# Attention by whole batches in 32-column tiles, with long-run loads, inside a fused attention and MoE kernel

## The reference

```python
def sm_attn(qq, kk, vv):
    s = scale * np.matmul(qq, kk.transpose(0, 1, 3, 2))
    s = s - np.max(s, axis=-1, keepdims=True)
    a = np.exp(s)
    a = a / (np.sum(a, axis=-1, keepdims=True) + 1e-09)
    return np.matmul(a, vv)
p_packed = sm_attn(p, k, v)            # 32 rows attend to 576
out = sm_attn(q, p_packed, p_packed)   # 576 rows attend to 32
...
k = np.maximum(xk @ w_k, 0.0); v = k * k @ w_v        # 512 -> 1024 -> 512
r = 1.0 / (1.0 + np.exp(-(xr @ w_r)))                 # xk, xr: x mixed with its previous row
x = r * v
...
u = x + (x^T @ U @ V)^T
out = u + np.maximum(u @ w_ch1, 0.0) @ w_ch2          # 512 -> 2048 -> 512
```

## Time and profile before

| | us |
|---|---|
| median of three runs | 1520.62 (1519.82 to 1520.99) |
| the profiled execution | 1520.71 |
| its span | 1518.4 |
| busy: PE / PE weight loads / DVE / ACT / POOL | 1449.3 / 1194.2 / 579.6 / 442.9 / 29.6 |
| granted TensorE clock, mean | 0.982 |

### The profile page before, as it was taken

One profiled execution on the slowest core, in us unless ns is written; L12 is line 12 of the kernel. 1 busy time (PEld: TensorE's weight loads), 2 busy tenths in 40 slices (PEclk: granted clock), 3 DMA queues, 4 the chain that ended last, 5 costly groups with the idle time before them and its releaser, 6 DMA issues.

```text
span 1518.4 us, 18053 instructions
## 1 busy us (share of the span) xinstructions
PE 1449.3 (95%) x7048; PEld 1194.2 (79%) x7048; DVE 579.6 (38%) x933; ACT 442.9 (29%) x766; POOL 29.6 (2%) x65
## 2 busy tenths in 40 slices
PE   3289999999999999999999999999999999999999
PEld 1177788888878878888888888888888888888887
DVE  3655766666666666535221221212112121121211
ACT  2353554554455445434211111111111111111110
POOL 5000000000000000000000000000000000000000
PEclk9599999999999999999999999999999999999999
DMA  9533343343233310035110010100101010010000
GB/s 212 148 70 76 77 90 77 80 84 84 69 88 72 87 46 20 21 104 182 52 55 8 0 63 0 63 1 15 48 0 63 1 57 6 1 56 0 29 0 28
DMA packets 144127, 84.90 MB, mean 56 GB/s; under 512 B 115440, under 2 KB 119696, under 8 KB 144048
## 3 DMA queue, kind: packets, MB, share of 16 engines
q1 hardware_dynamic: 142960, 82.51, 20.9%
q0 software_dynamic: 1088, 1.33, 0.5%
HBM read 63.36 MB, written 20.45 MB: 55 GB/s over the span
## 4 chain that ended last, share of the span: by engine, by line
PE 91%; DVE 3%; SPq 3%; issue 1%; ACT 1%; DMA 1%; DVEq 0%; ACTq 0%
PE bank L1058 26%; PE bank L1028 26%; PE bank L578 19%; PE bank L612 12%; SPq L823 1%; PE bank L678 1%; PE bank L404 1%; SPq L834 1%; PE bank L745 1%; PE bank L425 1%; PE bank L417 1%; PE bank L389 1%; DVE mixed L553 1%; PE bank L749 1%; PE bank L1044 1%
## 5 line engine op out<-in xcount | busy, mean ns | idle before, releaser
L1208 DVE SCALAR_TENSOR_TENSOR hid_lo<-bank,hid_hi 128x512 fp32r<-128x512 f32 x144 | 99.6, 692 | 499.3 <-ACT hid_hi L1138 499.3
L1138 ACT ACTIVATE hid_hi<-bank 128x512 fp32r<-128x512 f32 x144 | 86.1, 598 | 599.7 <-PE bank L1058 599.7
L1058 PE MATMUL bank<-uT_hi,w_hi 128*128 128x512 f32 x576 | 224.9, 390 | 0.0
L1058 PE MATMUL bank<-uT_hi,w_lo 128*128 128x512 f32 x576 | 224.4, 390 | 0.0
L1058 PE MATMUL bank<-uT_lo,w_hi 128*128 128x512 f32 x576 | 224.4, 390 | 0.0
L1028 PE MATMUL bank<-w_hi,hid_lo 128*128 128x512 f32 x576 | 224.2, 389 | 0.0
L1028 PE MATMUL bank<-w_hi,hid_hi 128*128 128x512 f32 x576 | 224.1, 389 | 0.0
L1028 PE MATMUL bank<-w_lo,hid_hi 128*128 128x512 f32 x576 | 224.1, 389 | 0.0
L578 PE MATMUL bank<-xk_hi,wk_hi 128*128 128x384 f32 x384 | 133.6, 348 | 3.7 <-DVE xk_lo L570 3.7
L578 PE MATMUL bank<-xk_lo,wk_hi 128*128 128x384 f32 x384 | 130.2, 339 | 0.0
L578 PE MATMUL bank<-xk_hi,wk_lo 128*128 128x384 f32 x384 | 130.2, 339 | 0.0
(11 more groups left out here) (152 smaller groups left out, 1722.0 us busy)
## 6 DMA issues: line engine op xcount, KB each, us to landing
k_parts<-in_k SPq DMA_DIRECT2D x60, 280.0 KB, 4.9
x_scratch<-x SPq DMA_DIRECT2D x36, 256.0 KB, 2.0
x_b<-x_scratch SPq DMA_DIRECT2D x9, 1024.0 KB, 6.2
out_dram<-x_b SPq DMA_DIRECT2D x36, 256.0 KB, 2.0
q_parts<-in_q SPq DMA_DIRECT2D x120, 72.0 KB, 2.3
x_b<-in_moe_w_ch SPq DMA_DIRECT2D x16, 512.0 KB, 3.9
v_rows<-in_v SPq DMA_DIRECT2D x120, 40.0 KB, 1.9
v_rows<-in_v SPq DMA_DIRECT2D x120, 32.0 KB, 1.8
```

The lines of the kernel that those rows point to most:

```text
L1058: last = nc.tensor.matmul(bank, w1s[a][:, ct, f * P:(f + 1) * P], uT[C % 2][b][:, ct, :], start=(ct == 0 and a == 0 and b == 0), stop=(ct ...
L1138: nc.scalar.activation(hid[0][:, f % RH, :], h_bank[(NFB * C + f) % 3], ACT.Relu).then_inc(h_hi, 1)
L1208: nc.vector.scalar_tensor_tensor(hid[1][:, f % RH, :], h_bank[(NFB * C + f) % 3], 0.0, hid[0][:, f % RH, :].bitcast(F32), ALU.max, ALU.sub ...
```

## The change

A batch's eight heads are now done together. There are no units and no side buffers, only `att` (class `Attention`). Heads 2c and 2c+1 (c = 0 to 3) lie on partition halves hp = 0, 1.

- `kqT` [128, 4, 576] holds k^T, then q^T, then the transposed second probabilities. It is filled by eight turns (i = 0 to 3 for k, 4 to 7 for q) on DVE, two in each of the steps kA, kB, qA, qB. A k turn is two transposes (512 and 64 columns).
- The source of turn i is `z[:, i % 2]`, with runs of 4480 bytes for k and q alike, loaded by four DMAs of 140 KB. There are two such buffers; batch 0 has six more early ones.
- p is loaded with its halves on partition quarters, scaled by POOL, and transposed by DVE; PE's step p, the mask and the block matrices go.
- v is loaded by six DMAs per batch with 1024-byte runs.
- PE's steps work on smaller tiles, for all eight heads. x has `outA` and `outB`, each for half of the tokens.
- The weights have three buffers instead of four, in other memory; the first mix needs batch 0 alone and no weights. DVE still does the low parts of the splitting.
- The middle loop is unrolled (Python `range` in place of `eng.Fori`).

```diff
-VLOADS = 16
+VLOADS = 6
+KQ = 2 * (DM // P)
+ZS = 2
-RA, RB = 4, 3
+RA, RB = 3, 3
-WEIGHTS_AFTER = {"a": 2, "pv": 2, "pp": 1, "scores2": 2, "norm": 3}
+WEIGHTS_AFTER = {"qB": 2, "pp": 2, "scores2": 2, "norm": 2, "outB": 2}
-def unit_slots(start, gaps=(0, 1, 2, 3, 4, 5, 6, 7, 8, 10, 11)):
-    steps = (("k",), ("p",), ("scores1",), ("q",), ("a",), ("pv",), ("pp",), ("scores2",), ("norm",), (), ("out",))
+def batch_slots(start, gaps=(0, 2, 3, 4, 5, 7, 8, 9, 11, 13, 17, 19)):
+    steps = (("kA",), ("kB", "p"), ("scores1",), ("qA",), ("a",), ("qB",), ("pv",), ("pp",), ("scores2",), ("norm",),
+             ("outA",), ("outB",))
...
+def batch_plans(kind):
+    if kind == FIRST:
+        early = {0: ("scores1",), 1: ("qA", "a"), 2: ("qB", "pv"), 3: ("pp",), 4: ("scores2",), 6: ("norm",),
+                 8: ("outA",), 9: ("outB",)}
+        return [(1, early), (2, batch_slots(14)), (3, batch_slots(31))]
+    return [(2, batch_slots(2)), (3, batch_slots(26))] if kind == MIDDLE else []
+
+LOADS_AFTER = {"kA": ("load_z", 0, 1), "kB": ("load_z", 0, 2), "qA": ("load_z", 0, 3), "qB": ("load_z", 1, 0),
+               "p": ("load_p", 1), "pv": ("load_v", 1)}
...
+    items += [("mix", 0, 0), ("split", 0, 0), ("attn", 1, "kA"), ("load_z", 1, 1), ("attn", 1, "kB"), ("load_z", 1, 2),
+              ("attn", 1, "p"), ("load_p", 2)]
```

A step's loads are issued one slot later. In FIRST, chunk 0, mix and split of xr still stand after slots 5 and 6, behind that slot's attention step. The waits and the loads:

```diff
+            eng.wait_ge(att.kq_ok, ZS if n == 1 and part == 0 else KQ * n + 2 * part)
+            for i in range(2):
+                load_z(eng, n, 2 * part + i)
...
+        for quad in range(4):
+            hp, dh = quad // 2, quad % 2
+            src = (k if i < CT else q)[n, 2 * (i % CT) + hp, :, :].rearrange("(i m) d -> i (m d)", m=KB)
+            eng.dma_start(part[32 * quad:32 * quad + 32, 0:KB * D - 32],
+                          src[:, 32 * dh:32 * dh + KB * D - 32]).then_inc(done, 16)
```

PE's steps (waits for earlier results as before, left out where they are plain):

```diff
+        if step == "scores1":
+            pe.wait_ge(L.pT_ok, n + 1)
+            pe.wait_ge(L.kq_ok, KQ * n + CT)
...
+            for h in range(2):
+                for c in range(CT):
+                    for hp in range(2):
+                        last = nc.tensor.matmul(L.reg[hp][quarter(c), h * 512:h * 512 + HALF],
+                                                L.pT[half_of(hp), c, :],
+                                                L.kqT[half_of(hp), c, h * HALF:(h + 1) * HALF], start=True, stop=True)
...
+            for hp in range(2):
+                for t in range(TT):
+                    for c in range(CT):
+                        last = nc.tensor.matmul(L.reg[0][quarter(c), half_of(hp)],
+                                                L.probs[:, hp, t * P + c * NP:t * P + (c + 1) * NP],
+                                                L.vn[:, 2 * c + hp, t, :], start=(t == 0), stop=(t == TT - 1))
...
+            for c in range(CT):
+                for hp in range(2):
+                    last = nc.tensor.matmul(L.reg[c // 2][half_of(hp), c % 2 * 512:c % 2 * 512 + HALF],
+                                            L.pk[quarter(c), hp, :],
+                                            L.kqT[quarter(c), hp, h * HALF:(h + 1) * HALF], start=True, stop=True)
```

More of the change, by code:

```diff
@@ L48 @@
 EPS = 1e-9
[L53 to L56, removed]
+UNIT_STEPS = ("kA", "kB", "p", "scores1", "qA", "a", "qB", "pv", "pp", "scores2", "norm", "outA", "outB")
 SLOTS = ([("k", f) for f in range(NFA)] + [("r", t) for t in range(TPC)]
@@ L304, in build @@
     flat = lambda t: t[:, :, :].rearrange("p b n -> p (b n)")
[L305 removed]
+    att.reg = [flat(t) for t in psum[:2]]
     moe_bank = [psum[2][:, 0, :], psum[2][:, 1, :], psum[3][:, 0, :]]
@@ L398, in pe_attn @@
         elif step == "pv":
[L399 removed]
+            pe.wait_ge(L.aT_ok, 2 * n + 2)
             pe.wait_ge(L.v_in, VLOADS * 16 * (n + 1))
[L401 to L405 removed]
@@ L430, in act_attn @@
-    def act_attn(act, L, n, place, step, mixes):
-        b, quad = place
-        if step == "p":
-            act.wait_ge(L.t_ps, NT * n + 1)
-            nc.scalar.activation(L.pT[:, :], L.reg_t[:, 0:P], ACT.Copy, scale=SCALE).then_inc(L.t_sb, 1)
-        elif step == "scores1":
-            act.wait_ge(L.s_sb, NS * n + 1)
-            nc.scalar.activation(L.probs[:, 0:S].rearrange("p (a n) -> p a n", a=2), halves(L.reg_s), ACT.Exp,
-                                 bias=L.neg_max[:, :], accum_out=L.row_sum[:, :]).then_inc(L.exp1, 1)
+                for c in range(CT):
+                    for hp in range(2):
+                        last = nc.tensor.matmul(L.reg[hp][quarter(c), h * 512:h * 512 + HALF],
+                                                L.pkT[half_of(hp), quarter(c)],
+                                                L.kqT[half_of(hp), c, h * HALF:(h + 1) * HALF], start=True, stop=True)
@@ L440, in act_attn @@
+    def act_attn(act, n, slot, step, mixes):
+        L = att
+        if step == "scores1":
+            for hp in range(2):
+                act.wait_ge(L.max1, 2 * n + hp + 1)
+                nc.scalar.activation(L.probs[:, hp, 0:S].rearrange("p (a n) -> p a n", a=2), halves(L.reg[hp]),
+                                     ACT.Exp, bias=L.neg_max[:, hp:hp + 1],
+                                     accum_out=L.row_sum[:, hp:hp + 1]).then_inc(L.exp1, 1)
         elif step == "a":
-            act.wait_ge(L.t_ps, NT * n + 2)
@@ L788, in everything @@
                 do_a(item, 0, c)
-        with eng.Fori(1, PAIRS - 1) as g:
+        for g in range(1, PAIRS - 1):
             for c in range(CHUNKS):
@@ L841, in _, with load_attn @@
+    def load_attn(eng, kind, n, part):
+        if n == B:
+            return
+        if kind == "load_p":
+            load_p(eng, n)
+        elif kind == "load_v":
+            load_v(eng, n)
+        else:
+            eng.wait_ge(att.kq_ok, ZS if n == 1 and part == 0 else KQ * n + 2 * part)
+            for i in range(2):
+                load_z(eng, n, 2 * part + i)
     @block.sync
```

506 lines of the change are left out of this document (235 added, 271 removed).

## The result

The changed kernel takes 1545.64 us (median of 4 runs, 1541.92 to 1548.79), the kernel before took 1520.8 beside it: ratio 1.0158, 95% interval 1.013 to 1.0187. It is slower by 1.6%, inside the range given, but 21.7 us over the time that was forecast.

A forecast was written before the change was run, and what follows sets the result against it. TensorE, busy nearly without a break, was taken to bound the first phase. Prologue 69.5, first pair 190.3, middle pairs 306.4, last pair 135.5, second phase 819.9 and 2.3 around the span gave 1523.9 us, range 1500 to 1554.

The forecast's parts named there:

- PE's share: TensorE's attention work: 8.2 us a batch instead of 12.5, saving 4.3; seven batches beside the MoE, -30 us.
- (c): Slower rival: small matmuls on PE bound by their number, 57 ns each, +27, 1551 us; chance 0.15.
- (d): Slower rival: more than two PE tiles don't overlap, 8.5 us more a batch, 1583 us; chance 0.07.
- main case: Whole kernel: PE and prologue gains outweighed by new waits, 1523.9 us, own range 1513 to 1534; chance 0.47.
- (b): Faster rival: chunk 0's links overlap DVE's passes (41 instead of 51 us), pv at its low end, 1507 us; chance 0.17.
- Chunk 0: First pair's first chunk: serial z loads and DVE's queue delay r0 to about X+51.4; 28 us lost, 1.5 slow clock.
- Middle pairs: Two middle pairs: 153.2 us each, with 4.9 us lost waiting for kB at scores1 and 1.5 of slow clock.
- Last pair: Last pair of batches: without a unit, 141.7 less 6.2, 135.5 us.
- Prologue: Start to first MoE group: last weight loaded after the seventh is split, PE starts at 69.5 us, -4 (+-5).
- Chunks 1 and 2: Rest of the first pair (190.3 us in all): batches 2 and 3 wait for kB at scores1, 6.8 us together.
- costed at nothing: Items given no cost, among them DVE's passes: as many per batch as two units', its 99 us stay.
- (a): Faster rival: z parts land sooner, each link 5.8 us instead of 8, 23 us less, 1501 us; chance 0.14.

The follow-up runs named there:

- e9: Changed kernel plus four half-size z buffers, early xr split, five weight buffers, and first-pair batches 2 and 3 reslotted with norm ahead of the mixes: 1501.3 us.
- e5: Changed kernel with only matmul order altered: pv runs five blocks of one column tile in a row, scores2 both halves of one tile: 1557.0 us.
- e2: Changed kernel with chunk 0's second mix and xr split moved ahead of scores2 (slot 1), batch 1's outs to slots 11 and 12: 1541.5 us.
- e3: Changed kernel with the middle pairs' first batch spread, its steps behind kA up to scores2 one to three slots later: 1542.6 us.
- e4: Changed kernel with five staging buffers instead of three for the prologue's weights: 1542.4 us.
- e10: As e9, with norm split into two half steps in slots of their own: 1495.5 us.
- e1: Changed kernel with first-pair batch 3's kA moved behind batch 2's outB (slot 31 to 34), its following steps drawn together: 1545.2 us.
- e12: As e11, with the change's two long-run z buffers put back and batch 1's first part asked for behind kB: 1527.5 us, ratio 1.0051 to before.
- e11: The e10 kernel again, timed in rounds against the kernel before: 1494.78 us, ratio 0.9828.
- e6: Changed kernel with four half-size z buffers instead of two, loaded in 128-byte runs after the first four parts: 1529.2 us.

## Why the prediction was right and where it was wrong

**PE's share: right, and under-sized.** scores1, scores2 and the transposes cost 1.13, 1.13 and 1.01, as said; pv 1.25 instead of 2.2, the low bound; an out 0.67. In e9's middle pair, at a clock of 1.00, PE is busy 143.5 us against 153.9: 5.2 a batch, where 4.3 was forecast. Rivals (c) and (d) fall with these rows, though (c)'s 1551 lies nearer to the measured time than the main case's: e5 shows what pv costs tile by tile, 3.23 us. Rival (b) is half right: pv is at its low end, chunk 0 is not shorter. The Trainium skill's 62 ns for every matmul without hardware decoding ("TensorE: Matmul & The Clock Gate", Wait, 56ns, not 53.3ns?) is four times what the 16 ns of pv show.

**Chunk 0: right, in its parts too.** With X = 75.75, the start of the first k group, scores1 starts at X + 9.1 (forecast: X + 9.8 for kB), pp at X + 27.0 (28.1), the split of xr is done at X + 51.5 (51.4) and r0 starts at X + 51.7. The chain of the changed kernel (start us, us) has these places:

```profile
84.89 2.18 PE bank L385 x32
...
102.73 0.47 PE bank L408
...
125.63 1.65 DVE xr_lo L603 x2
```

Beyond PE's own work, put at 23.2 us, 28.5 are lost to r0 (28 forecast, slow groups included). In the trace 22.0 of them are waits (4.96 at scores1, 4.81 at pp, 12.27 at r0); the first, second and fifth k groups take 4.18, 4.01 and 4.12 us instead of 2.09, 6 us more together. The forecast had the first two of these slow and the third not. Behind the last wait r0 takes 5.02 us, where an r group beside a small step takes 2.85: 2.2 of slow clock against 1.5. e2 shows the wait for xr_lo to be the order that the forecast described.

**Middle pairs: right, in part by luck.** 154.3 and 153.5 against 153.2, with 4.2 and 4.4 us at scores1 (4.9 forecast). But PE's own work was counted at 146.3 and is 143.5 (e9), and PE idles 8.2 us in each pair and not 4.9: 2.0 at a k group, behind norm on DVE, 0.8 at outA and some smaller waits were not in the forecast. The two offset each other. e3 took the waits at scores1 away, and 4 to 4.6 us with them. **Last pair:** 133.9 against 135.5.

**Prologue: wrong by 6.3.** 75.75 instead of 69.5. The failed step is "the last one is loaded only after the seventh is split": it looked at the last weight only. With three buffers the fourth is already asked for late (34.88), behind the 1.1 MB of a z part and beside v, and DVE stands 5.5 us for it. The last one, which the forecast had loaded at about 57, is asked for at 64.4. e4 gives the 69.96.

**Chunks 1 and 2: wrong by 17, and this is the main miss.** The forecast's 190.3 less 51.4 to r0 and the 29.4 that the chunk takes behind r0 leaves 109.5 us; they took 126.6. The step that failed is the one costed at nothing: "DVE's passes per batch are as many as two units', so its 99 us stay". The sum nearly stays (426.3 us over the first phase against 419.2 in the earlier trace rows), but not its grain: norm of a batch is a block of 6.5 us in an in-order queue, where it was two of 2.7 in slots of their own, and in the first pair its slots 27 and 44 are the mixes' (26 to 31, 43 to 48). What stands behind a long item had been counted for the z links, and not for norm; the links themselves cost less here than forecast (3.7 us at scores1 against 5.0). e9 gives 14.5 us of these two chunks back, less the 2.6 that go to chunk 0, and e10 another 6.7, with no work taken off DVE; e10 does it by norm's grain and slots alone, e9 by these together with 5.3 us less on ACT. ACT is not in the forecast's account at all: with scores2's exponentials between its sigmoids it kept DVE waiting 4.15 and 3.77 us just ahead of norm. The kernel before has 10 table loads in its first pair, one more than the changed one, so it is their place and not their number that can count; how much of the 17 us it is was not measured. That kA's wait for the outB of batch 2 was overlooked as well seems to count for less: 7.2 us in the trace, 0.7 in e1, which also moved norm.

The deviation adds up: prologue 6.3, first pair 17.4, middle pairs 1.4, last pair -1.6, together 23.5 us of span, the forecast's 1521.6 against 1545.1.

Rival (a) asked for a part in 5 us. The chain of the changed kernel in chunk 0 (start us, us) has 6.7 from the first issue to the last part's turn, against the forecast's 7.0, so (a) falls:

```profile
77.10 0.34 SPq L846
...
83.81 0.71 DVE kqT L484
```

## What to carry to other kernels

Fusing two units of work into one saves on the engine that is the bound and coarsens the grain on the others: list every block of more than a few microseconds that an in-order queue now holds, and who asks for what stands behind it; halve or move these first. Look at each in-order queue that a stage passes through, ACT's as well as DVE's. Twice the buffers with short runs were worth more than long runs once transfers run beside other work (behind the prologue 38 us at slots fitted to them, e12 against e11, and 25 at the change's own slots, e6), and cost 5.6 to 7.5 us in a prologue that waits for bytes. Taking away a stall with a clean releaser can bring next to nothing (e1, 0.7 us for a wait of 4.1): what is late next decides, so look at the block before the stall too.

## What the runs showed of the hardware

- 80 matmuls of 128x32 tiles with 64 columns take 1.25 us going round four column tiles and 3.23 us tile by tile; 32 of 64x32 with 288 columns take 1.13 and 1.18 us in the two orders tried.
- The 32x32-block transpose of 128x576 on DVE takes 1258 ns where it writes with a stride of 18 elements (L539) and 779 ns where the kernel before wrote it in a row (L507).

```profile
L539 DVE STREAM_TRANSPOSE kqT<-probs 128x576 f32<-128x576 f32 x16 | 20.1, 1258 | 0.6
```

- Loads of 32 partitions in runs of 128 B (72 KB) land after 2.7 us (median, e6), the same rows in long runs (140 KB) after 3.2 (the changed kernel).
- In chunk 0 the k group behind each of the waits of 4.96 and 4.81 us takes 4.01 and 4.12 us instead of 2.09. In the wait of 12.27 us for xr_lo the granted clock falls from 1.00 to 0.50 (from 2.4 to 1.2 GHz), and it is still 0.50 when r0 starts (0.50 in the mean from 118.31 to 131.90 us), which takes 5.02 us instead of 2.85. What in the wait brings it down was not tried.
- ACT_TABLE_LOAD takes 1.28 us, and the trace has one wherever ACT goes from the exponential to the sigmoid or back: 9 in the first pair of the changed kernel, 5 in e9, where the exponentials were moved together.
